# The last 64 rows' low-by-high terms of two column tiles as two 64-row matmuls, in a fused linear-attention and two-layer network kernel

## The reference, cut to what matters

```python
x = np.ascontiguousarray(attn_out.transpose(0, 2, 1, 3)).reshape(B * S, H * D)
# first layer: d_model 320, d_ff 2048
h = x @ w_in
g = np.maximum(h, 0.0) + alpha * np.minimum(h, 0.0)
x = (g @ w_out).astype(np.float32)
# second layer: d_ff 768
h = np.maximum(np.maximum(x @ w1, x @ w2), x @ w3)
return (h @ w_out).astype(np.float32)
```

## Time and profile before

| | |
|---|---|
| time, median of 3 runs | 805.46 us (802.93 to 806.68) |
| profiled execution, first to last instruction | 803.0 us |
| TensorE busy | 754.5 us (94%) |
| VectorE busy | 541.9 us (67%) |
| ScalarE busy | 298.8 us (37%) |
| GpSimd busy | 206.7 us (26%) |
| L597, hidden matmuls | 1024 of 384 columns |
| chain that ended last | PE 70%, DVE 20% |

### The profile page before, as it was taken

How to read it: one execution, slowest core, us unless ns; L and a number is a source line. 1 busy time by engine, 2 the same in 40 slices (tenths; PEclk the granted TensorE clock), 3 DMA queues, 4 the chain that set the end, 5 groups by cost and what they waited for, 6 DMA issues and landing times.

```text
span 803.0 us, 13943 instructions
## 1 busy us (share of the span) xinstructions
PE 754.5 (94%) x4658; PEld 702.0 (87%) x4658; DVE 541.9 (67%) x870; ACT 298.8 (37%) x685; POOL 206.7 (26%) x206
## 2 busy tenths in 40 slices
PE   1659999999999999999999999699999999999997
PEld 1649999999999999999999998698888888888886
DVE  7697997997997997997988985934243342434222
ACT  3535436436436436436435435331211212121211
POOL 5382432432433333333333312700000000000000
PEclk9968999999999999999999999999999999999999
DMA  6970321321311212222210009011020202000000
GB/s 197 279 236 18 119 69 41 118 67 46 113 67 62 97 67 82 77 67 89 70 67 24 0 0 283 6 39 65 1 72 1 72 0 72 0 33 1 33 1 33
DMA packets 37145, 55.93 MB, mean 70 GB/s; under 512 B 3329, under 2 KB 27458, under 8 KB 36738
## 3 DMA queue, kind: packets, MB, share of 16 engines
q1 hardware_dynamic: 36690, 54.57, 21.1%
q10 hardware_dynamic: 432, 1.06, 0.5%
HBM read 47.65 MB, written 7.96 MB: 69 GB/s over the span
## 4 chain that ended last, share of the span: by engine, by line
PE 70%; DVE 20%; issue 5%; DMA 1%; ACT 1%; SPq 1%; DVEq 0%; POOL 0%; ACTq 0%
PE bank L640 25%; PE bank L597 16%; DVE scale L936 4%; PE bank L613 4%; DVE g_lo L953 4%; PE bank L615 4%; PE bank L614 3%; PE bank L533 3%; PE bank L653 3%; PE bank L654 3%; PE bank L655 3%; DVE g_full L965 2%; PE bank L618 2%; PE bank L617 2%; DVE inner L910 2%
## 5 line engine op out<-in xcount | busy, mean ns | idle before, releaser
L597 PE MATMUL bank<-x_split,w_hi 128*128 128x384 f32 x640 | 182.9, 351 | 0.7 <-ACT x_split L738 0.7
L597 PE MATMUL bank<-x_split,w_lo 128*128 128x384 f32 x384 | 130.7, 340 | 0.0
L597 PEld LDWEIGHTS bank<-x_split,w_hi 128*128 128x128 f32 x640 | 119.1, 191 | 2.9 <-DVE g_full L965 1.8
L953 DVE TENSOR_TENSOR g_lo<-g_full,g_hi 128x384 fp32r<-128x384 f32 x128 | 104.7, 818 | 23.1 <-ACT g_hi L773 22.1
L773 ACT ACTIVATE g_hi<-g_full 128x384 fp32r<-128x384 f32 x128 | 66.6, 520 | 133.9 <-DVE g_full L965 133.9
L613 PE MATMUL bank<-g_hi,wproj 128*128 128x384 f32 x256 | 94.7, 370 | 8.9 <-DVE g_lo L953 8.1
L757 ACT ACTIVATE g_full<-bank 128x384 f32<-128x384 f32 x128 | 62.5, 488 | 99.2 <-PE bank L597 99.1
L1002 DVE TENSOR_TENSOR best<-bank,first_of_max 128x512 f32<-128x512 f32 x36 | 24.9, 692 | 108.1 <-PE bank L640 81.3
L965 DVE SCALAR_TENSOR_TENSOR g_full<-g_full,beta,bank 128x384 f32<-128x384 f32 x128 | 77.8, 608 | 17.5 <-ACT g_full L757 17.5
L615 PE MATMUL bank<-g_hi,wproj 128*128 128x384 f32 x256 | 87.0, 340 | 0.0
L614 PE MATMUL bank<-g_lo,wproj 128*128 128x384 f32 x256 | 86.7, 339 | 0.0
(11 more groups left out here) (115 smaller groups left out, 1506.1 us busy)
## 6 DMA issues: line engine op xcount, KB each, us to landing
u_bcast<-u_scratch SPq DMA_DIRECT2D x24, 512.0 KB, 4.3
kvo<-in_kvo SPq DMA_DIRECT2D x24, 484.0 KB, 3.5
out<-final SPq DMA_DIRECT2D x6, 640.0 KB, 3.4
layer_scratch<-rows SPq DMA_DIRECT2D x8, 384.0 KB, 2.4
q_t<-in_q_t SPq DMA_DIRECT2D x24, 120.0 KB
k_t<-in_k_t SPq DMA_DIRECT2D x48, 60.0 KB
wproj_raw<-in_w_out SPq DMA_DIRECT2D x1, 2560.0 KB, 16.7
w_raw<-in_w_max SPq DMA_DIRECT2D x2, 1152.0 KB, 9.7
```

Of the source, the lines that this page charges most:

```text
L597: ins = pe.matmul(ps[:, 0:T], w[:, a, f], xs[:, x, :], start=(m == 0), stop=(m == 7))
L953: dve.tensor_tensor(gl[:, j % G_SLOTS, :], gf[:, j % GF_SLOTS, :], gh[:, j % G_SLOTS, :].bitcast(F32), ALU.subtract).then_inc(g_lo_done, 1)
```

## The change

Column tiles go in pairs. A new step `halves` j (j even) stands ahead of hidden j and hidden j + 1. It issues two matmuls of 64 contraction rows each: the low weights' rows 0 to 63 for tile j into bank 0, and rows 64 to 127 for tile j + 1 into bank 1. Each starts the accumulation in its bank; the hidden steps then have 7 matmuls instead of 8. Since both banks are written, `halves` waits for `hid_read` of n + 2, so for tile j-1 too. For rows 64 to 127 the high part of x must stand in those rows, so `x_split` gets a sixth tile, which ScalarE fills: its one activation in `turn` becomes three.

```diff
-    moe = [("hidden", 0), ("hidden", 1)]
-    for j in range(J1 - 2):
-        moe += [("hidden", j + 2), ("project", j)]
-    head, tail = moe[:-1], [("project", j) for j in (J1 - 3, J1 - 2, J1 - 1)]
+    moe = [("halves", 0), ("hidden", 0), ("hidden", 1)]
+    for j in range(0, J1 - 2, 2):
+        moe += [("halves", j + 2), ("hidden", j + 2), ("hidden", j + 3), ("project", j), ("project", j + 1)]
+    moe = moe[:-1]
+    head, tail = moe, [("project", j) for j in (J1 - 3, J1 - 2, J1 - 1)]
...
-                if kind == "hidden":
+                if kind == "halves":
...
-                    pe.wait_ge(hid_read, n + 1)
+                    pe.wait_ge(hid_read, n + 2)
+                    low = slice(j * 128, (j + 1) * 128)
+                    up = slice((j + 1) * 128, (j + 2) * 128)
+                    pe.matmul(hid[0][:, 0:T], w1l[0:64, 2, low], xs[0:64, 2, :], start=True, stop=False)
+                    pe.matmul(hid[1][:, 0:T], w1l[64:128, 2, up], xs[64:128, 5, :], start=True, stop=False)
+                if kind == "hidden":
...
                     terms = [(w1h, 0, 0), (w1l, 0, 0), (w1h, 1, 1), (w1l, 1, 1), (w1h, 0, 3), (w1h, 1, 4),
-                             (w1h, 2, 2), (w1l, 2, 2)]
+                             (w1h, 2, 2)]
...
-                        ins = pe.matmul(ps[:, 0:T], w[:, a, f], xs[:, x, :], start=(m == 0), stop=(m == 7))
+                        ins = pe.matmul(ps[:, 0:T], w[:, a, f], xs[:, x, :], start=False, stop=(m == 6))
...
-                    act.activation(xs[:, 0:3, c * L:(c + 1) * L], ps[:, 0:3 * L].rearrange("p (a t) -> p a t", a=3),
-                                   ACT.Copy).then_inc(x_high, 1)
+                    t = slice(c * L, (c + 1) * L)
+                    act.activation(xs[:, 0:2, t], ps[:, 0:2 * L].rearrange("p (a t) -> p a t", a=2), ACT.Copy)
+                    act.activation(xs[0:64, 2, t], ps[0:64, 2 * L:3 * L], ACT.Copy)
+                    act.activation(xs[64:128, 5, t], ps[64:128, 2 * L:3 * L], ACT.Copy).then_inc(x_high, 1)
...
-                    dve.tensor_tensor(xs[64:128, 2, t], src[64:128, 2, :], xs[64:128, 2, t].bitcast(F32),
+                    dve.tensor_tensor(xs[64:128, 2, t], src[64:128, 2, :], xs[64:128, 5, t].bitcast(F32),
```

More of the change, by code:

```diff
@@ L97 @@
 TASK_STEPS = [s for s in plan() if s[0] in ("scores", "carry", "state", "values", "turn")]
-LAYER1 = ("hidden", "project", "rows_out")
+LAYER1 = ("halves", "hidden", "project", "rows_out")
 PLAN = plan()
@@ L188, in build @@
         beta, _ = sb("beta", [128, J1], F32)
-        xs, xs_at = sb("x_split", [128, 5, T], F32R)
+        xs, xs_at = sb("x_split", [128, 6, T], F32R)
         gf, _ = sb("g_full", [128, GF_SLOTS, T], F32)
```

## The result

| | before | changed |
|---|---|---|
| time, median | 804.48 us (802.93 to 806.68, 4 runs) | 852.44 us (849.7 to 854.31, 4 runs) |
| ratio | | 1.059 (95% interval 1.056 to 1.062) |
| profiled execution, first to last instruction | 803.0 us | 852.4 us |
| first layer, first to last matmul step | 60.77 to 534.66 | 60.90 to 584.04 |

The change costs 48 us, twice what was forecast, and just over the top of the range. Nearly all of it lies in the first layer: 473.9 us before, 523.1 after; layer two took 268.3 and 268.4.

What follows compares the result with a forecast made beforehand. TensorE's packed stream was taken as the bound. Terms 19.2 + 1.4 + 1.8 + 4.5 + 1.4 - 5.5 = +22.8 us on the 803.0 span gave 825.8; with 2.5 for the median, 828 us, 2.8% slower, 8-in-10 range 814 to 852.

Steps and rivals of the forecast that it cites:

- The wait at a block's start: TensorE at `halves` 2 waits for VectorE's read of tile 1: 3.2 us at each of 6 loop boundaries, 19.2 us.
- The pairs' price: On TensorE, each of 64 pairs saves 0.175 us less 0.09 for one exposed weight load: 5.5 us gained.
- the worst end: Pessimistic bound for a pair on TensorE: the array empties before and after, 0.155 us lost per pair, 9.9 in all.
- The clock: TensorE at half clock behind block-start waits: 1.5 us at half of the 6 loop boundaries, 4.5 us, ends 0 and 9.
- First and last block: TensorE's block-start wait outside the 6 loop boundaries: 1.4 us in the first block, 1.8 us in the last.
- The waits around GpSimd's passes: Last block: VectorE's four long low parts stay and start later; counted at nothing, give or take 3 us.
- The middle of a block: Pairs needing both tiles read while VectorE is busy mid-block: 0.2 us for each of 7 iterations, 1.4, ends 0 and 7.
- The `finish` cover: Mid-block, projects and attention steps hide a tile's 2.8 us chain despite VectorE's long `finish` work; 1.4 us allowed.
- The three copies: ScalarE's three activations in `turn` instead of one: about 0.45 us more, covered by project 15, cost nothing.
- "drains": Rival: TensorE's array drains at each shape change, each pair loses 0.155 us; 843 to 844 us, chance 0.21.
- "Paid back": Rival: the block-start wait replaces later TensorE waits behind `finish`, only saved places count; 800 us, at best 794, chance 0.06.

## Why the prediction was wrong, point by point

The direction and the cause of the largest part were right; the sum was 22.8 on the span and came out at 49.4. By the lengths of the blocks and the steps in them that is waits 17.1, pairs 12.8, clock 11.8, first and last block 6.8 and turns 0.9, where 19.2, -5.5, 4.5, 3.2 and 1.4 (for the middle of the blocks) were forecast. The steps:

- **The wait at a block's start: right.** 3.2 us were forecast for each of six boundaries; 2.85 were measured (19.2 against 17.1), with the instructions in the order that was written down. Two small errors met there: the chain took 5.90 from the block's start and not 6.02, and TensorE came 0.23 later, by the first pair's own price. The experiment without 64-row matmuls shows that the wait comes from the order and the second bank alone, and the one with the gates moved that 0.75 of it is the gate.
- **The pairs' price: the step that failed, and with the wrong sign.** I took one exposed weight load, 0.09, and a gain of 5.5. The halves do overlap (same start; 0.17 longer when they can't), but a stay in the 64-row shape costs 0.41 in full: the loads of the pair and of the matmul behind it both start late, and two longer places go with each, so each pair loses 0.2 in the mean of a block, 8 x 8 x 0.2 = 13 us in all. That is 18 of the 27 us that were missing. The bound was also too tight: I had put the worst end at 0.155 a pair; one read in full is 0.23. The sentence of the Trainium skill, page "TensorEngine Tiling (Array Packing)", section "Key Properties", that a change of tiling mode drains TensorE fits the traces as far as they go: each change of shape costs time on both sides of it (0.10 to enter, 0.12 behind), but no row shows the array empty. What the Trainium skill says of matmuls of different row groups, page "TensorE: Matmul & The Clock Gate", Part 3, agrees with them (same start). Both hold at once; I had let them stand against each other and chosen between.
- **The clock: the mechanism right, the size off.** I gave half of the six boundaries 1.5. All six fell, 1.5 each, and two of them 1.4 more: 11.8 in place of 4.5. That is another 7.3.
- **First and last block.** 1.4 and 1.8 were forecast beside the pairs; by the length of the blocks it was 3.0 (66.17 against 61.53, less 1.6 for pairs) and 3.8 (61.5 against 56.1, less 1.6). The waits were 1.87 and 1.68; the rest was again low clock behind them (granted 0.66 in both). The waits around GpSimd's passes, which I had set at nothing, give or take 3, came to 7.6 in three against 8.1 in five before. But the clock was low behind two of them (0.54 and 0.66 in the 5 us from there), where it had been low behind one.
- **The middle of a block: 1.4 forecast, under 1 measured,** and that in the turns: no pair there waited. The `finish` cover held. It did not hold, for instance, where the order left one project between a tile and the next pair (the old order with pairs: 0.67 and 0.48).
- **The three copies: right**, nothing, and measured by themselves.

Of the rivals, "drains" was the one on the array, and it came together with the forecast wait; its 843 to 844 lacked the clock, and 2.9 of the pairs (12.8 against 9.9). "Paid back" fell: no variant with pairs had a block under 61.9 us, where the old one takes 59.4.

## What to carry to other kernels

Cost a new shape on the matrix engine as a fixed price for each stay (here 0.41 us, more than two 384-column matmuls), and bring enough into one stay to pay it: with 0.18 for each pair and 0.35 saved, an estimate from these numbers is that only three pairs in one stay would win (0.95 against 1.05), which needs six banks. When an edit makes one step need two buffers, look for the place in the list where nothing stands between the last reader and that step, and build the chain there from the old rows with the queues in their new order. And where a wait of some microseconds is put into a dense matmul stream, count a slow stretch behind it as the likely case, here 1.5 us: it came behind 21 of the 30 waits of 2.0 to 3.2 us in the loops of five kernels.

## What the runs showed of the hardware

- Entering and leaving the 64-row shape cost 0.10 and 0.12 us and held the pair for 0.37 instead of 0.175, whether one or two matmuls ran in it. At each change the weight load started with its own matmul, and not with the one ahead of it.
- The clock after a wait did not go by the wait's length. 3.18 us (the order alone): low behind all six in the loop. 2.79: low behind all six. 2.04: low behind all six. 2.62: low behind two of six. 2.6 in the kernel with doubled pairs: low behind one of six. And 2.61 low, 2.41 not, in the kernel before; at the last block's start 1.68 low in the changed kernel, 1.67 not in the one with both halves in the same rows. Where a wait falls in time differs from kernel to kernel, so what decides may be where in time the wait falls; no run was made that shifts it alone, and this stays open. It moved whole experiments: two variants with more array work took no or only 2 us more than the changed kernel, since fewer of their waits were followed by half clock. Only the distances in the trace, not the times, told the theories apart there.
- With GpSimd busy on a pass over 2304 columns, a subtraction of 384 columns on VectorE took 5.2 us instead of 0.56, and 0.56 again with the pass gone.
